# Later outputs, later normalisings and six turns in one group, in an mLSTM and mixture-of-experts kernel

## The chip, the cores and the metric

The kernel runs on one core of a Trainium2 chip. The metric is the device time of one execution in microseconds (us). Before the change it is 632.3 us, the median of three runs (631.77 to 632.38). The profiled execution took 632.11 us, of which the profile's span covers 630.3.

Names: PE is TensorE (matrix products), DVE is VectorE, ACT is ScalarE, POOL is GpSimd, SP is SyncE, which issues most of the DMAs. SBUF is the memory of the engines, PSUM the small one into which PE writes.

## The reference

Three stages in a row, all in fp32:

```python
# 1: mLSTM, batch 2, heads 8, sequence 768, head size 40 -> y (B,H,S,D)
m_new = max(f_gate + m, i_gate); f = exp(f_gate + m - m_new); i = exp(i_gate - m_new)
C = f*C + i*outer(v, k); n = f*n + i*k
y[t] = sigmoid(o_gate) * (C q) / max(|n.q|, 1)
# 2: four experts on x = y as (1536, 320), all of them for every token
out = sum_e p[:, e] * (relu(x @ w1[e]) @ w2[e])        # w1 320x1024, w2 1024x320
# 3: gated product
out = ((x @ w_a) * (x @ w_b)) @ w_out                  # 320x1536, 1536x320
```

## The kernel before, in words

**Stage 1** works in 12 units `u` of 128 tokens (6 chunks of time by 2 batches). For each unit PE multiplies queries and keys (`products`), reads the state (`from_state`), and multiplies the weighted scores with the values (`outputs`, 16 matmuls of 41 columns). DVE weighs the scores (`weigh`), scales the part from the state, takes the numerator out of PSUM (`take_num`), and normalises it: three operations on a tile `den` of 8 columns and one product into `normed` (`normalise`). POOL multiplies that with the output gate into `acc` (`gate_output`, which increments the semaphore `x_ready`). One bank holds the outputs of a unit, so `outputs(u)` waits until `take_num(u-1)` is done. In the last units PE also multiplies ones by ones (`keep_busy`), results of which nobody reads.

**Stages 2 and 3** work in 56 groups `n`. A group takes one pair of blocks of 128 hidden columns and one half of the tokens (768 of them). Its first layer is a two-by-two block product done with seven products instead of eight, on sums and differences of blocks of weights and of x (the operand of x has seven pieces, made of four quarters `raw` by four `x_sum` steps). Each product stands for fp32 as a high and a low part in a rounded format: PE issues four matmuls of 384 columns per product, high by high, high by low, low by high, and the remaining rows. ACT makes the high parts (`x_high`, `high_a`, `high_s`, `high_w2`, `high_hidden`), DVE the low parts by subtraction (`x_low`, `low_w2`, `low_relu`), POOL those of the weights. Groups 0 to 31 are the experts (eight groups an expert: four for one half of the tokens, four for the other), 32 to 55 the gated product.

Two PSUM banks, A and B, take the seven products in turn, so the steps of a group hang together: product 0 to A, `keep_p1` (ACT) copies it, product 1 to B, `make_c11` (DVE) adds the two; product 2, copied by `keep_u2`; product 3 needs c11 made; product 4, copied by `keep_w`; product 6 needs `make_c22` (B plus that copy); `make_c12` ends the group. PE fills in between with the second layer of the group before (36 matmuls of 320 columns in an expert's group, in portions given by `chunks`, the function `between` issues one portion after each product and each turn). The next group's product 0 waits for the second `low_relu` of this one, its product 1 for `make_c12`.

**Turning.** x is transposed by PE, 128 tokens at a time: six turns give one half of the tokens. Set 0 is turned during stage 1; sets 1, 2 and 3 (`BASES`, the group from which each is made ready) within groups. ACT first replicates a tail of 32 columns (`replicate`), PE turns `acc` and tail into bank B (`turn`), ACT copies the bank to `raw` (`keep_turned`), and only then can bank B be used again. When six are kept, the seven pieces of the operand are made (`x_high`, `x_low`, `x_sum`) for the half that starts at group 4, 32 or 36. Before, groups 1 and 2 turn three each for set 1, 29 and 30 for set 2, 33 and 34 for set 3.

**Order.** Each engine has its own written order and takes its instructions strictly in that order; semaphores hold an instruction until its inputs are there, and with it all behind it on its engine. Group 0 has no second layer to fill in, so there `between` issues the outputs of the last unit (half behind product 0, half behind product 1) and then 13 products with the identity (`keep_warm`).

Some tiles of the groups lie where tiles of stage 1 were. So ACT's `high_a(2)` and `high_a(3)`, the high parts of the third and fourth block of weights, wait until all twelve units have been gated:

```python
elif p >= 2:
    act.wait_ge(x_ready, NU)          # L633, in high_a
```

Of the kernel before, what the change touches and what calls it, by code (L numbers as in the profile page):

```python
# [26 lines left out]
P = 128  # L27
# [26 lines left out]
def mlstm_moe_kernel(nc, qk_t, tok, gates, late, probs, wt, wtail, w2, w_out, out):  # L54
    with ExitStack() as ctx:
# [159 lines left out]
        TURNS_AFTER = {0: (0,), 2: (1, 2)}  # L215

# [173 lines left out]
        def _(pool):  # L390
# [101 lines left out]
            for u in range(NU):  # L492
# [4 lines left out]
                if u >= 1:  # L497
                    sigmoid(u - 1)
                    gate_output(u - 1)
# [47 lines left out]
        def _(act):  # L547
# [231 lines left out]
            def keep_turn(n, k):  # L779

                if turning(n) is not None:
                    s, first = turning(n)
                    keep_turned(s, first + k, B_BANK)

            def expert_group(n):
# [7 lines left out]
                replicate_late(b2, 5)  # L793
                if b2 is not None:
                    x_high(b2, 0)
                high_c11(n)
                keep_u2(n)
                keep_turn(n, 1)
                keep_turn(n, 2)
                if b2 is not None:  # L800
                    x_high(b2, 1)
                if b3 is not None:
                    x_high(b3, 3)
# [5 lines left out]
                if n == 0:  # L809
                    prepare_weights(n)  # L810
                replicate_late(b1, 3)
                if b2 is not None:
                    x_high(b2, 2)
                if b3 is not None:
                    x_high(b3, 4)
# [5 lines left out]
                replicate_late(b1, 4)  # L821
                if b3 is not None:
                    x_high(b3, 5)
# [43 lines left out]
        def _(dve):  # L867
# [158 lines left out]
            for u in range(NU):  # L1026
# [5 lines left out]
                if u >= 1:  # L1032
# [3 lines left out]
                    normalise(u - 1)  # L1036
                if u >= 7:
                    x_low(0, u - 7)
                if u == 11:
                    low_w2(0)  # L1040
# [73 lines left out]
            def expert_group(n):  # L1114

                p = n % NP1
                b2, b3, b4 = (set_at(n, k) for k in (2, 3, 4))
                if p == 1:
                    add_tiles(n, range(HB, UB))
                if n == 0:  # L1120
                    x_low(0, 5)
                make_c11(n)
                if n == 0:
                    x_low(0, 6)
                    take_num(NU - 1)
                    normalise(NU - 1)
                low_relu(n, 0, c11_s[:, :])
# [366 lines left out]
```

## Time and profile before

| | before |
|---|---|
| median of three runs | 632.3 us (631.77 to 632.38) |
| the profiled execution | 632.11 us |
| its span | 630.3 us |
| PE busy in the span | 614.3 us (97%) |
| PE weight loads | 590.1 us (94%) |
| DVE busy | 375.2 us (60%) |
| ACT busy | 300.2 us (48%) |
| POOL busy | 221.6 us (35%) |
| mean granted clock of PE | 0.989 of full speed |

Stage 1 ends and group 0 begins at 79.00 us in the span; the gated groups begin at 424.79. "Idle before" in a row is the time for which the engine stood still ahead of an instruction, with the instruction that ended the wait. PE's matmuls overlap in the rows, so that the distance from start to start is what one costs. PEclk is the clock granted to PE, 1.00 for 2.4 GHz and 0.50 for 1.2 GHz; in a row of a longer stretch it is the mean.

### The profile page before, as it was taken

To read this page: it belongs to the slowest core of one execution; us is meant where nothing else is said; L and a number is where in the kernel's file an instruction comes from. 1 tells how busy PE (TensorE), PEld (TensorE's weight loads), DVE (VectorE), ACT (ScalarE), POOL (GpSimd) and SP (SyncE) were. 2 spreads that over 40 slices of the span, in tenths; PEclk is the share of its full clock that TensorE was granted. 3 is DMA by queue.
4 is the path that set the end of the run, shared out by engine and by line. 5 is a ranking of instruction groups with operands and counts; after the bars stand their busy time and mean duration, and the time that the engine had idled before them with its cause. 6 is when DMAs were issued, how large, how long until landed. Compare 5 with 4: busy or idle time off the path is not lost. (4 is left out here: it accounts for less than half of the span.)

```text
span 630.3 us, 11170 instructions
## 1 busy us (share of the span) xinstructions
PE 614.3 (97%) x4035; PEld 590.1 (94%) x4045; DVE 375.2 (60%) x714; ACT 300.2 (48%) x644; POOL 221.6 (35%) x289
## 2 busy tenths in 40 slices
PE   7999989999999999999999999999989999999997
PEld 6888889999999999999999999988779999999997
DVE  7577985685364353644444535387597564757565
ACT  4778645654444344443445434645644443444332
POOL 3468774032530033500435101364244640464000
PEclk9999959999999999999999999999999999999999
DMA  3667505102041002310022100113100420030011
GB/s 121 194 213 190 152 4 171 38 1 46 23 131 56 4 13 55 120 49 22 2 66 82 55 12 2 45 35 90 35 11 8 121 75 11 19 71 2 0 63 64
DMA packets 21063, 38.98 MB, mean 62 GB/s; under 512 B 3600, under 2 KB 11312, under 8 KB 21008
## 3 DMA queue, kind: packets, MB, share of 16 engines
q1 hardware_dynamic: 18976, 35.57, 20.1%
q10 hardware_dynamic: 2032, 2.68, 1.5%
q8 instruction: 33, 0.54, 0.4%
q14 instruction: 22, 0.18, 0.1%
HBM read 26.42 MB, written 1.97 MB: 45 GB/s over the span
## 5 line engine op out<-in xcount | busy, mean ns | idle before, releaser
L1386 PE MATMUL PS<-w2h,hh 128*128 128x320 f32 x528 | 164.5, 311 | 0.2
L1386 PE MATMUL PS<-w2l,hh 128*128 128x320 f32 x528 | 164.1, 311 | 0.0
L1386 PE MATMUL PS<-w2h,hl 128*128 128x320 f32 x528 | 163.2, 309 | 0.0
L1362 PE MATMUL PS<-xop,wop 128*128 128x384 f32 x392 | 139.2, 355 | 7.5 <-DVE xop L875 3.1
L670 ACT ACTIVATE hh<-c_s 128x384 fp32r<-128x384 f32 x144 | 75.3, 523 | 130.1 <-DVE c_s L1074 43.6
L1365 PE MATMUL PS<-xop,wop 96*128 96x384 f32 x392 | 133.0, 339 | 0.0
L1363 PE MATMUL PS<-xop,wop 128*128 128x384 f32 x392 | 132.8, 339 | 0.0
L1364 PE MATMUL PS<-xop,wop 128*128 128x384 f32 x392 | 132.7, 339 | 0.0
L1067 DVE TENSOR_TENSOR c_s<-PS,w_s 128x384 f32<-128x384 f32 x56 | 31.2, 558 | 122.9 <-ACT w_s L688 88.4
L1386 PEld LDWEIGHTS PS<-w2h,hh 128*128 128x128 f32 x528 | 99.5, 189 | 1.4 <-DVE hl L1051 1.2
L1386 PEld LDWEIGHTS PS<-w2l,hh 128*128 128x128 f32 x528 | 99.7, 189 | 0.0
L1386 PEld LDWEIGHTS PS<-w2h,hl 128*128 128x128 f32 x528 | 99.5, 188 | 0.0
L1362 PEld LDWEIGHTS PS<-xop,wop 128*128 128x128 f32 x392 | 74.2, 189 | 17.9 <-DVE xop L875 5.1
L452 POOL TENSOR_TENSOR wop<-s,wop 128x512 fp32r<-128x512 f32 x28 | 36.6, 1306 | 134.1 <-ACT wop L638 134.1
L1045 DVE SCALAR_TENSOR_TENSOR hl<-c_s,hh 128x384 fp32r<-128x384 f32 x96 | 56.2, 586 | 41.7 <-ACT hh L670 41.7
L1363 PEld LDWEIGHTS PS<-xop,wop 128*128 128x128 f32 x392 | 74.4, 190 | 0.0
L1365 PEld LDWEIGHTS PS<-xop,wop 96*128 96x128 f32 x392 | 74.2, 189 | 0.0
L1364 PEld LDWEIGHTS PS<-xop,wop 128*128 128x128 f32 x392 | 74.1, 189 | 0.0
L688 ACT ACTIVATE w_s<-PS 128x384 f32<-128x384 f32 x56 | 27.5, 491 | 80.5 <-PE PS L1365 80.4
L471 POOL TENSOR_TENSOR t1l<-t,t1h 128x384 fp32r<-128x384 f32 x7 | 7.1, 1019 | 115.1 <-ACT t1h L644 115.1
L1060 DVE TENSOR_TENSOR c_s<-PS,p_s 128x384 f32<-128x384 f32 x56 | 31.0, 554 | 21.3 <-PE PS L1365 21.1
L447 POOL TENSOR_TENSOR wop<-s,wop 128x384 fp32r<-128x384 f32 x28 | 29.5, 1052 | 39.8 <-ACT wop L634 39.8
(137 smaller groups left out, 866.0 us busy)
## 6 DMA issues: line engine op xcount, KB each, us to landing
wop<-t1h SPq DMA_DIRECT2D x56, 112.0 KB, 2.2
s<-in_wt SPq DMA_DIRECT2D x24, 256.0 KB, 3.0
kvo<-in_tok SPq DMA_DIRECT2D x12, 480.0 KB, 4.8
qk<-in_qk_t SPq DMA_DIRECT2D x24, 160.0 KB
s<-in_w SPq DMA_DIRECT2D x12, 320.0 KB, 3.0
wop<-t1l SPq DMA_DIRECT2D x28, 112.0 KB, 2.2
s<-in_w_out SPq DMA_DIRECT2D x12, 160.0 KB, 2.2
out_y<-acc SPq DMA_DIRECT2D x12, 160.0 KB, 1.9
```

The source lines that it names most:

```text
L447: nc.gpsimd.tensor_tensor(wop[p][:, 2, 0:3 * P], s1[:, p, P:4 * P], f32(wop[p][:, 0, 0:3 * P]), ALU.subtract).then_inc(w_lo_a, 1)
L452: nc.gpsimd.tensor_tensor(wop[p][:, 2, 3 * P:7 * P], s1[:, p, :], f32(wop[p][:, 0, 3 * P:7 * P]), ALU.subtract).then_inc(w_lo_s, 1)
L670: nc.scalar.activation(hh[:, home(n, k), :], src, ACT.Relu if n < FIRST else ACT.Copy).then_inc(hh_ready, 1)
L688: nc.scalar.activation(w_s[:, :], PS[:, A_BANK, 0:HT], ACT.Copy).then_inc(w_kept, 1)
L1045: nc.vector.scalar_tensor_tensor(out=hl[:, home(n, k), :], in0=src, scalar=0.0, in1=f32(hh[:, home(n, k), :]), op0=ALU.max, op1=ALU.subtra ...
L1060: nc.vector.tensor_tensor(c11_s[:, :], PS[:, B_BANK, 0:HT], p1_s[:, :], ALU.add).then_inc(c11_made, 1)
L1067: nc.vector.tensor_tensor(c22_s[:, :], PS[:, B_BANK, 0:HT], w_s[:, :], ALU.add).then_inc(c22_made, 1)
L1362: nc.tensor.matmul(bank, ws[0], xs[0], start=opens, stop=False, skip_group_check=True)
L1363: nc.tensor.matmul(bank, ws[0], xs[2], start=False, stop=False, skip_group_check=True)
L1364: nc.tensor.matmul(bank, ws[2], xs[0], start=False, stop=False, skip_group_check=True)
L1365: nc.tensor.matmul(bank, ws[1][0:96, :], xs[1][0:96, :], start=False, stop=closes, skip_group_check=True).then_inc(prod_done, 1)
L1386: got = nc.tensor.matmul(bank, left, (w2l if part == 1 else w2h)[p][:, f, :], start=opens and part == 0, stop=closes and part == 2)
```

## The change

Six edits, most of them to the order in which an engine has its instructions:

1. `keep_busy` in units 7 to 11 has two products of ones for three.
2. Group 0: both halves of the last unit's outputs now stand behind product 1. The identity products are ten for thirteen, go to another bank (`keep_fed`) and stand in portions of 2, 0, 1, 1, 2, 2, 2.
3. DVE: `normalise` of units 10 and 11 moves from ahead of the first `low_relu` of group 0 to the end of group 0, one ahead of `make_c12`, one behind it. The low parts 4, 5 and 6 of x stand together behind `make_c11`, `low_w2(0)` behind `make_c22`, `low_w2(1)` and the weights of the experts in group 1.
4. POOL: the x sum 2 moves from unit 10 to unit 9; the last two gates behind the sums and low parts of the second block of weights. ACT: `prepare_weights(0)`, which issues `high_a(2)`, moves to the end of group 0.
5. The six turns of set 1 are all in group 1, those of set 2 all in group 29: one behind product 0, five behind product 2. Set 3 stays as it was.
6. `x_high`, `x_low`, `x_sum` of sets 1 and 2 move about one group forward; the replication of the tails with them, in group 29 one ahead of `keep_u2` and two between kept turns.

```diff
+            for s in (1, 2):
+                if n == BASES[s] + 1:
+                    return s, 0, UB
             for part in range(2):
-                if set_at(n, part + 1) is not None:
-                    return set_at(n, part + 1), HB * part
+                if n == BASES[3] + 1 + part:
+                    return 3, HB * part, HB
...
+        def turns_behind(n, i):
+            if turning(n) is None or i not in (0, 2):
+                return ()
+            return (0,) if i == 0 else range(1, turning(n)[2])
...
-                return (3, 6, 1, 0, 6, 6, 1, 6, 4, 3) if n <= FIRST else (0, 5, 1, 0, 4, 4, 0, 3, 1, 0)
+                return (0, 5, 1, 0, 4, 5, 5, 4, 4, 1, 4, 1, 2) if n <= FIRST else (0, 5, 1, 0, 4, 4, 0, 3, 1, 0)
@@ POOL @@
-                    gate_output(u - 1)
+                    if u < NU - 1:
+                        gate_output(u - 1)
...
-                if u in (8, 9, 10):
+                if u in (8, 9):
                     x_sum(0, u - 8)
+                if u == 9:
+                    x_sum(0, 2)
                 if u == 10:
                     x_sum(0, 3)
+            sums(1)
             sigmoid(NU - 1)
-            sums(1)
+            low_s(1)
+            gate_output(NU - 2)
             gate_output(NU - 1)
-            low_s(1)
@@ ACT, expert_group @@
                 high_c11(n)
+                replicate_late(b1, 3)
                 keep_u2(n)
                 keep_turn(n, 1)
+                replicate_late(b1, 4)
                 keep_turn(n, 2)
...
+                replicate_late(b1, 5)
+                for k in range(3, UB):
+                    keep_turn(n, k)
...
                 keep_w(n)
-                if n == 0:
-                    prepare_weights(n)
...
                 replicate_late(b0, 1)
...
+                if n == 0:
+                    prepare_weights(n)
@@ DVE, units @@
-                    normalise(u - 1)
-                if u >= 7:
+                    if u < NU - 1:
+                        normalise(u - 1)
+                if 7 <= u < NU - 1:
                     x_low(0, u - 7)
@@ DVE, expert_group @@
                 low_relu(n, 2, c22_s[:, :])
+                if n == 0:
+                    normalise(NU - 2)
                 make_c12(n)
+                if n == 0:
+                    normalise(NU - 1)
                 low_relu(n, 3, c12_s[:, :])
@@ PE, between @@
-                    if slot < 2:
-                        outputs(NU - 1, (slot,))
+                    if slot == 1:
+                        outputs(NU - 1)
                     else:
-                        keep_warm((2, 3, 4, 2, 2)[slot - 2])
+                        keep_fed((2, 0, 1, 1, 2, 2, 2)[slot])
...
-                    keep_busy(3)
+                    keep_busy(2)
```

DVE in group 0, from the last low part of x (`xop0`) on; `num`, `den` and `normed` are the last units' tiles, `hl` the low parts of the hidden tile. Before:

```order
L874 TENSOR_TENSOR xop0<-raw,xop0 128x384 [waits x_hi]
L875 TENSOR_TENSOR xop0<-raw,xop0 32x384
L936 TENSOR_TENSOR num1<-PS,inter_s1 128x328 [waits inter_scaled,pv_done]
L944 SCALAR_TENSOR_TENSOR den1<-num1 128x8 [waits num_ready]
L946 TENSOR_SCALAR den1<-den1 128x8 [waits den_ready]
L948 RECIPROCAL den1<-den1 128x8 [waits den_ready]
L952 TENSOR_TENSOR normed1<-num1,den1 128x320 [waits den_ready,x_ready]
L1045 SCALAR_TENSOR_TENSOR hl<-c11_s,hh 128x384 [waits hh_ready]
L1067 TENSOR_TENSOR c22_s<-PS,w_s 128x384 [waits w_kept,prod_done]
L1045 SCALAR_TENSOR_TENSOR hl<-PS,hh 128x384 [waits hh_ready]
L1045 SCALAR_TENSOR_TENSOR hl<-c22_s,hh 128x384 [waits hh_ready]
```

And now, from `low_w2(0)` on:

```order
L903 TENSOR_TENSOR w2l0<-s2,w2h0 128x640 [waits w2_hi]
L1057 SCALAR_TENSOR_TENSOR hl<-PS,hh 128x384 [waits hh_ready]
L1057 SCALAR_TENSOR_TENSOR hl<-c22_s,hh 128x384 [waits hh_ready]
L957 SCALAR_TENSOR_TENSOR den0<-num0 128x8 [waits num_ready]
L959 TENSOR_SCALAR den0<-den0 128x8 [waits den_ready]
L961 RECIPROCAL den0<-den0 128x8 [waits den_ready]
L965 TENSOR_TENSOR normed0<-num0,den0 128x320 [waits den_ready,x_ready]
L1086 TENSOR_TENSOR c12_s<-PS,u2_s 128x384 [waits u2_kept,prod_done]
L957 SCALAR_TENSOR_TENSOR den1<-num1 128x8 [waits num_ready]
L959 TENSOR_SCALAR den1<-den1 128x8 [waits den_ready]
L961 RECIPROCAL den1<-den1 128x8 [waits den_ready]
L965 TENSOR_TENSOR normed1<-num1,den1 128x320 [waits den_ready,x_ready]
```

One normalising stood ahead of the first low part of `hl` (the other further up, in unit 11); now two stand around the c12 sum, behind the third.

ACT from group 0's `high_s(1)` (`wop1`) to group 1's first kept turn (`raw`); `wop2` is `high_a(2)`, `p1_s` is group 1's `keep_p1`. Before:

```order
L638 ACTIVATE wop1<-s1 128x512 [waits w_sum]
L688 ACTIVATE w_s<-PS 128x384 [waits prod_done]
L634 ACTIVATE wop2<-s1 128x384 [waits x_ready,w_in2]
L670 ACTIVATE hh<-PS 128x384 [waits prod_done]
L670 ACTIVATE hh<-c22_s 128x384 [waits c22_made]
L670 ACTIVATE hh<-c12_s 128x384 [waits c12_made]
L676 ACTIVATE p1_s<-PS 128x384 [waits c11_made,prod_done]
L583 ACTIVATE raw<-PS 128x2x2x128 [waits x_lo,xt_done]
```

And now:

```order
L649 ACTIVATE wop1<-s1 128x512 [waits w_sum]
L699 ACTIVATE w_s<-PS 128x384 [waits prod_done]
L681 ACTIVATE hh<-PS 128x384 [waits prod_done]
L681 ACTIVATE hh<-c22_s 128x384 [waits c22_made]
L681 ACTIVATE hh<-c12_s 128x384 [waits c12_made]
L645 ACTIVATE wop2<-s1 128x384 [waits x_ready,w_in2]
L687 ACTIVATE p1_s<-PS 128x384 [waits c11_made,prod_done]
L594 ACTIVATE raw<-PS 128x2x2x128 [waits x_lo,xt_done]
```

`high_a(2)`, with its wait for all twelve gates, moved from ahead of the group's last three high parts of `hh` to right ahead of group 1's `keep_p1` and kept turn.

## Rows read from the trace of the kernel before

**Rows 1.** Page, busy time by engine: us, share of the span, instructions.

```profile
PE 614.3 (97%) x4035; PEld 590.1 (94%) x4045; DVE 375.2 (60%) x714; ACT 300.2 (48%) x644; POOL 221.6 (35%) x289
```

**Rows 2.** Windows by stage: stretch, its length, busy us by engine, granted clock, DMA.

```profile
79.00:96.92 17.92, 16.04 (x73) 15.48 (x72) 14.11 (x25) 7.18 (x16) 14.02 (x17) 0.62 0.11 26
96.92:121.03 24.11, 24.10 (x156) 22.80 (x154) 14.26 (x26) 15.37 (x32) 6.74 (x8) 1.00 0.35 106
121.03:143.00 21.97, 21.16 (x130) 20.37 (x129) 18.57 (x32) 9.78 (x19) 5.79 (x7) 1.00 0.06 16
143.00:153.18 10.18, 10.18 (x66) 10.18 (x65) 5.05 (x11) 4.25 (x9) 4.12 (x6) 1.00 0.01 2
388.58:412.66 24.08, 24.05 (x154) 22.66 (x153) 12.07 (x22) 16.11 (x39) 7.72 (x10) 1.00 0.13 30
412.66:436.84 24.18, 21.46 (x131) 20.42 (x130) 19.54 (x31) 11.73 (x26) 11.80 (x13) 1.00 0.25 69
```

**Rows 3.** The same view by the microsecond, where the granted clock changes.

```profile
81.00:82.00 1.00, 0.91 (x5) 0.94 (x5) 0.97 (x2) 0.73 (x1) 1.00 (x2) 0.54 0.00 0
...
94.00:95.00 1.00, 1.00 (x7) 1.00 (x6) 0.37 (x1) 0.12 (x1) 1.00 (x2) 0.64 0.59 136
```

**Rows 4.** Timeline of PE: start, us, line, operation, count, idle before.

```profile
77.26 1.92 PE L1290 MATMUL PS<-vx,pt 128*128 128x41 f32 x16
...
79.00 0.42 PE L1362 MATMUL PS<-xop,wop 128*128 128x384 f32 x1
...
81.09 1.90 PE L1290 MATMUL PS<-vx,pt 128*128 128x41 f32 x8 [1.13 <-DVE num L936]
...
85.77 0.67 PE L1362 MATMUL PS<-xop,wop 128*128 128x384 f32 x1
...
89.00 0.66 PE L1362 MATMUL PS<-xop,wop 128*128 128x384 f32 x1 [0.75 <-DVE c_s L1060]
...
91.55 0.67 PE L1362 MATMUL PS<-xop,wop 128*128 128x384 f32 x1
```

**Rows 5.** Timeline of POOL, then of DVE, then of POOL again.

```profile
78.25 4.38 POOL L489 TENSOR_TENSOR raw<-raw 128x384 f32<-128x384 f32 x4
...
80.87 0.84 DVE L944 SCALAR_TENSOR_TENSOR den<-num 128x8 f32<-128x8 f32 x1
...
84.31 1.10 DVE L875 TENSOR_TENSOR xop<-raw,xop 32x384 fp32r<-32x384 f32 x1
...
90.68 0.17 DVE L944 SCALAR_TENSOR_TENSOR den<-num 128x8 f32<-128x8 f32 x1
...
91.97 1.12 POOL L441 TENSOR_TENSOR acc<-normed,ogate 128x320 f32<-128x320 f32 x1 [2.85 <-DVE normed L952]
...
98.85 0.82 DVE L890 TENSOR_TENSOR w2l<-s,w2h 128x640 fp32r<-128x640 f32 x1
```

**Rows 6.** Timeline of ACT, then the page's groups of instructions (busy, mean ns).

```profile
83.42 0.47 ACT L676 ACTIVATE p_s<-PS 128x384 f32<-128x384 f32 x1
...
L670 ACT ACTIVATE hh<-c_s 128x384 fp32r<-128x384 f32 x144 | 75.3, 523 | 130.1 <-DVE c_s L1074 43.6
...
L1045 DVE SCALAR_TENSOR_TENSOR hl<-c_s,hh 128x384 fp32r<-128x384 f32 x96 | 56.2, 586 | 41.7 <-ACT hh L670 41.7
```

**Rows 7.** Timeline of PE and ACT in group 1.

```profile
99.45 0.43 PE L1362 MATMUL PS<-xop,wop 128*128 128x384 f32 x1
...
102.60 0.33 PE L1206 MATMUL PS<-identf,acc 128*128 128x128 f32 x1
...
103.29 0.60 ACT L583 ACTIVATE raw<-PS 128x512 f32<-128x512 f32 x1 [0.74 <-PE PS L1208]
...
104.03 0.41 PE L1362 MATMUL PS<-xop,wop 128*128 128x384 f32 x1
```

**Rows 8.** Timeline of PE at groups 31 and 32, the longest pauses.

```profile
424.79 0.41 PE L1362 MATMUL PS<-xop,wop 128*128 128x384 f32 x1 [0.89 <-DVE hl L1045]
...
429.26 0.45 PE L1362 MATMUL PS<-xop,wop 128*128 128x384 f32 x1 [1.52 <-DVE xop L875]
```

More of the change, by code:

```diff
@@ L214, in mlstm_moe_kernel @@
         BASES = {1: 0, 2: FIRST - NP1, 3: FIRST}
-        TURNS_AFTER = {0: (0,), 2: (1, 2)}
         def set_at(n, k):
@@ L779, in keep_turn @@
             def keep_turn(n, k):
-                if turning(n) is not None:
-                    s, first = turning(n)
+                if turning(n) is not None and k < turning(n)[2]:
+                    s, first, _ = turning(n)
                     keep_turned(s, first + k, B_BANK)
@@ L820, in expert_group @@
                 replicate_late(b0, 1)
-                replicate_late(b1, 4)
-                if b3 is not None:
-                    x_high(b3, 5)
+                if b1 is not None:
+                    x_high(b1, 1)
+                if b2 is not None:
+                    x_high(b2, 4)
+                if n == 0:
+                    prepare_weights(n)
             def gated_group(n):
@@ L1116, in expert_group @@
                 p = n % NP1
-                b2, b3, b4 = (set_at(n, k) for k in (2, 3, 4))
+                b1, b2, b3, b4 = (set_at(n, k) for k in range(1, 5))
                 if p == 1:
                     add_tiles(n, range(HB, UB))
-                if n == 0:
-                    x_low(0, 5)
                 make_c11(n)
                 if n == 0:
-                    x_low(0, 6)
+                    for k in (4, 5, 6):
+                        x_low(0, k)
                     take_num(NU - 1)
-                    normalise(NU - 1)
                 low_relu(n, 0, c11_s[:, :])
+                if n == 1:
+                    low_w2(1)
                 if b2 is not None:
-                    x_low(b2, 0)
                     x_low(b2, 1)
+                    x_low(b2, 2)
+                    x_sum(b2, 0)
                 if b3 is not None:
-                    x_low(b3, 3)
-                    x_sum(b3, 1)
+                    x_sum(b3, 2)
+                    x_low(b3, 4)
                 if b4 is not None:
-                    x_low(b4, 5)
                     x_low(b4, 6)
@@ L1139, in expert_group @@
                     add_tiles(n, range(HB))
-                if b3 is not None:
-                    x_sum(b3, 2)
+                if n == 0:
+                    low_w2(0)
+                if b2 is not None:
+                    x_sum(b2, 1)
                 w2_lows(n)
@@ L1215, in keep_busy, with keep_fed @@
                     nc.tensor.matmul(PS[:, INTER, BUSY_COLS:BUSY_COLS + P], ones[:, :], ones[:, :], start=True, stop=True)
-            def keep_warm(n):
-                pe.wait_ge(inter_scaled, NU - B)
+            def keep_fed(n):
+                pe.wait_ge(state_ready, 2 * OLD)
                 for _ in range(n):
-                    nc.tensor.matmul(PS[:, INTER, BUSY_COLS:BUSY_COLS + P], identf[:, :], identf[:, :], start=True, stop=True)
+                    nc.tensor.matmul(PS[:, UPD, BUSY_COLS:BUSY_COLS + P], identf[:, :], identf[:, :], start=True, stop=True)
             def log_weights(u):
@@ L1338, in product @@
                 if turning(n) is not None and i == 1:
-                    s, first = turning(n)
+                    s, first, _ = turning(n)
                     pe.wait_ge(raw_ready, UB * s + first + 1)
@@ L1349, in product @@
                     if turning(n) is not None:
-                        s, first = turning(n)
-                        pe.wait_ge(raw_ready, UB * s + first + 3)
+                        s, first, count = turning(n)
+                        pe.wait_ge(raw_ready, UB * s + first + count)
                 elif i == 4:
@@ L1409, in turn_within @@
             def turn_within(n, k):
-                s, first = turning(n)
+                s, first, _ = turning(n)
                 if k == 0:
@@ L1451, in _ @@
                     slot += 1
-                    for k in TURNS_AFTER.get(i, ()) if turning(n) is not None else ():
+                    for k in turns_behind(n, i):
                         turn_within(n, k)
```

30 lines of the change are left out of this document (13 added, 17 removed).

## The prediction

> **What bounds the kernel now.** I read first the page's list of engines: TensorE is busy for 97% of the span [rows 1], so a change pays only where TensorE stands still, runs at the low clock, or gets less to do. Then the busy times by stage [rows 2]. A plain group of the experts takes 10.18 us. Five stretches hold what the change touches. Group 0 (79.00 to 96.92) takes 17.92 us at a mean granted clock of 0.62. Groups 1 and 2, with three turns each, take 24.11 together; groups 29 and 30 take 24.08. Against two plain groups (20.36) that is 3.7 us, 0.62 a turn, with TensorE never idle. Groups 3 and 4 take 21.97, so 1.6 are lost there; groups 31 and 32 take 24.18, so 3.8 are lost. The biggest pauses of the latter are 0.89 us (for the first low part of the hidden tile) and 1.52 us (for a low part of x) [rows 8].
>
> Next, the clock by the microsecond [rows 3]: it falls to its half level, 1.2 GHz, in the microsecond from 81 and is back at 2.4 GHz within the one from 94, some 13.6 us later. TensorE's own timeline [rows 4] shows what was before the fall: product 0 at 79.00, then a pause of 1.13 us for the last but one `take_num`. The second pause, 0.75 us, is ahead of product 3 at 89.00, and the clock rises 5.7 us after it.
>
> **The change, part by part, in the profiled execution's time (632.11 us, of which 630.3 are the span; the median is 632.3, 0.2 more).**
>
> *Ones and identity.* Five units lose one product of ones and group 0 has 10 identity products for 13. Only the one in unit 11 stands behind the last wait; I value it at 0.3 us earlier for product 0. The rest is filler in waits: nothing.
>
> *x sums.* GpSimd now does the third x sum in unit 9, right behind the second, ahead of unit 9's gate and so beside `normalise(9)`. In unit 11 of before, with four such sub-operations running from 78.25 for 4.38 us (1.1 each), the small den operation at 80.87 takes 0.84 us, and at 90.68, with GpSimd idle, 0.17 [rows 5]. Each ended when the GpSimd operation beside it ended. So `normalise(9)` and all that DVE does behind it in order, weigh, scale and `take_num(10)`, come 1.1 us later: `take_num(10)` ends at 81.95 for 80.84. The Trainium skill, "SBUF — State Buffer", section "SBUF: two separate sides", has this as a rule: an operation of VectorE with two inputs in SBUF and one of GpSimd take the shared port pair exclusively for the whole instruction. The trace agrees (0.84 against 0.17); were the port merely shared in width, this 1.1 us would be nearly nothing and the forecast 1 us lower.
>
> *Group 0.* Product 1 follows product 0 and ends about 80.9; the outputs wait for `take_num(10)` until 82.2, a pause of 1.3 us in place of 1.13. They then take 1.74 us (77.26 to 79.00 at the full clock [rows 4]). ACT's queue ahead of `keep_p1` is unchanged in length and ends its copy at 83.9 as before [rows 6]: unit 11's gates start 1.1 us later, but the wait for the last x sum is gone. DVE has the first c11 sum now ahead of the low parts 4, 5 and 6: c11 at 84.0 to 84.5, low part 4, with contention like the 1.10 us at 84.31 [rows 5], to 86.2. Product 2 waits for it until 86.4 (85.77 before), a second pause of over 2 us. So the clock falls here again. From 86.4 TensorE is never idle. By columns of the plain group (28 matmuls of 384 and 36 of 320 in 10.18 us) a product of four matmuls takes 0.70 us and a second-layer matmul 0.146; at half rate a product takes 1.4, and 89.00 to 91.55 [rows 4] leaves 0.4 for each of three identity products. Product 4 ends near 91.4 (91.55 + 1.4 = 93.0 before). If the clock rises 5.7 us after the pause, as in [rows 3, 4], that is at 92.1; group 0 ends at about 94.2 instead of 96.92. The pause ahead of product 3 is gone.
>
> *What is late next.* That gain of 2.7 us is, I think, lost at once. DVE now has, behind c22 and the low part of w2 (0.82 us with GpSimd idle, at 98.85), two low parts of 0.5, `normalise(10)`, the c12 sum, `normalise(11)`. A normalising is 1.2 us (90.68 to the gate at 91.97) [rows 5]. In numbers from 91.4 (durations overlap their neighbours by some 0.1): w copied 92.0; c22 92.6; w2 93.3; two low parts 94.4 (pitch from 586 ns each, the first waits for ACT, 523 ns [rows 6]); normalise 95.5; c12 96.0; normalise 97.4 (it meets the gate of unit 10); gate of unit 11, 1.12 us, 98.55 at best. ACT has `high_a(2)` at the end of group 0, which waits for all twelve gates, and behind it in order stand `keep_p1(1)` and the first kept turn of group 1. High part, copy and kept turn (0.45 + 0.4 + 0.6) end at 100.05. Product 1 of group 1 waits for that kept turn: 100.1 for 99.45 [rows 7]. Of the 6 us before it TensorE works 2: product 0, one turn (behind c12, 96.0) and five second-layer matmuls. **Cost 0.65 us**, with pauses of 1.3 and 2.8 us where there was none. Bounds: -0.5 (no contention on the port and an early rise) to +1.6.
>
> *Clock in group 1.* A pause of 1.13 us beside light work was enough at 81; a pause of 1.52 at 427.7, in dense work, was not (mean clock 1.00 in that stretch [rows 2, 8]). With 4 us idle of 6 I take the clock to fall. By the 5.7 us of before it is back at about 105.8, at the earliest near 103.5. In that time products 1 and 2 and the first turn run at half rate: 1.7 us of work to product 2's end twice over, and 0.3 to 0.5 of the first turn's interval. **Cost 2.0 us**; bounds 0 (no fall) and 2.9.
>
> *Six turns in one group.* All use bank B, so each waits until ACT has copied the one before: turn at 102.60, copy from 103.29 for 0.60, next at 104.03, an interval of 1.43 with six second-layer matmuls in it [rows 7]. With four or five in it, it would be 1.0 to 1.2 for TensorE, but the copy still holds it at 1.3 to 1.43; I take 1.37. Five such intervals are 6.85 us with 22 matmuls; before, the five hold 30 and take some 7.2. Eight matmuls (1.2 us) are owed for 0.35 saved. Ahead of product 1, where turn and copy bind, five stand for nine: 0.6 owed. Together 1.45, less 0.1 to 0.2 of switches between kinds: **1.3 us** at group 1, and 0.1 for a late low part at the end. At group 29 ACT in addition replicates a tail ahead of `keep_u2` and of the kept turn, which puts turn 2 0.4 us later: **1.75 us**. Bounds for both together 1.5 to 4.
>
> *A group earlier.* All six turned, the operand of the next half is split from group 2 (30) on. DVE's work between c11 and c22 of the group before its use falls from two low parts' and two sums' worth to one of each, and only low part 6 is left to the group of its use, whose sum GpSimd has by then. Its last wait moves behind product 4. I give back all of the 1.6 us of groups 3 and 4 and the 3.8 of 31 and 32: **-1.6 and -3.8**; bounds -0.6 and -2 (in groups 2 and 30 DVE gets two low parts, two sums and, in group 2, a w2 low part ahead of the low part on which the next group waits).
>
> *Sum.* 0.65 + 2.0 + 1.4 - 1.6 + 1.75 - 3.8 = +0.4 us. 632.1 + 0.4 = 632.5, on the median's footing **632.7 us**.
>
> **Rivals.** (1) *The clock holds in group 1*: for it, a pause of 1.52 did nothing at 427.7; against it, 1.13 sufficed at 81. Then 632.7 - 2.0 = 630.7. (2) *The chain over both normalisings is shorter*: no contention in units 9 and 11, so product 1 of group 1 comes at 99, the pause ahead is below 2 us and the clock stays: 632.7 - 1.1 - 2.0 = 629.6. (3) *The prepared operand does not come earlier where it counts*: DVE falls behind in groups 2 and 30, its operations lengthened beside GpSimd by up to 0.7 us each (0.84 for 0.17 [rows 5]), and the low part of the hidden tile holds product 0 of the next group. It decides once DVE needs over 7 us from c11 to that low part (product 1's end to the next product 0 is 8 us in a plain group, less 1 for c11 and ACT). Of the 5.4 given back 2.0 stay lost: 634.7, slower. For it: DVE is the releaser of both pauses shown. Against: it is busy 19.54 of 24.18 us there [rows 2], so the order binds and not its load.
>
> **How the numbers follow.** The likeliest, with its own range of 631.6 to 633.9, gets 0.47; rival 1 0.2; rival 2 0.1; rival 3, with a clock that stays low for longer (up to 2.9), 0.23. What a measurement can tell from no change is 0.2%, 1.3 us: under 631.0 or over 633.6. Faster: 0.2 + 0.1 = 0.30. Slower: 0.23 and a fifth of the likeliest, 0.32. Same: 0.38. Range: 629.8 to 635.2, which leaves out half of rival 2 and a tail of rival 3.
>
> **What would show it.** The outputs of unit 11 behind product 1 with 1.2 us or so idle ahead; product 2 at 86 to 86.5; group 0 ended by 94 to 95; DVE's two normalisings at 94 to 97.5; ACT waiting for the gate on GpSimd; product 1 of group 1 at 100; the clock low a second time from about 98 to 105; turns 1.3 to 1.45 us apart; groups 3, 4, 31 and 32 at 10.2 each. I am wrong if group 1 starts before 94 and its product 1 before 99, if the clock is 1.00 from 95 on, or if groups 31 and 32 together still take over 22 us.

## The result, and the profile after

The changed kernel takes **641.42 us** (median, 640.54 to 642.33, 4 runs), the kernel before beside it 632.34 us (631.77 to 633.45, 4 runs): ratio **1.0142, 95% interval 1.012 to 1.0163**. It is 9.1 us slower; forecast were 632.7 us and a range of 629.8 to 635.2. The profiled execution took 642.33 us, the longest of the four, with a span of 640.5: its stages below add up to 10.3 us, and what they share out is this one execution's difference, 1.2 us more than that of the medians.

The page's line of engines answers to [rows 1]: TensorE's busy time is the same (614.3 before), so the 10 us of the span are time in which it stands, 26.4 us for 16.0.

```profile
PE 614.1 (96%) x4019; PEld 587.9 (92%) x4029; DVE 374.1 (58%) x714; ACT 301.0 (47%) x644; POOL 220.5 (34%) x289
```

Windows by stage show where. The first five rows answer to [rows 2] stretch by stretch (group 0; 1 and 2; 3 and 4; 29 and 30; 31 and 32), the last three are single groups: 2, 29 and 30.

```profile
79.02:94.97 15.95, 12.15 (x66) 11.66 (x66) 10.85 (x19) 7.44 (x17) 8.20 (x10) 0.79 0.00 1
94.97:130.44 35.47, 28.13 (x155) 24.81 (x154) 18.93 (x38) 16.72 (x34) 10.85 (x14) 0.90 0.30 85
130.44:150.89 20.45, 20.45 (x128) 20.45 (x129) 15.75 (x28) 9.26 (x18) 5.57 (x7) 1.00 0.06 17
396.46:426.00 29.54, 25.39 (x154) 22.57 (x153) 15.33 (x25) 17.05 (x40) 10.34 (x12) 1.00 0.11 25
426.00:447.12 21.12, 20.98 (x130) 20.48 (x129) 16.71 (x27) 11.23 (x25) 9.67 (x10) 1.00 0.28 78
117.51:130.44 12.93, 11.06 (x64) 10.20 (x65) 11.42 (x21) 6.55 (x12) 2.14 (x3) 1.00 0.16 47
396.46:413.75 17.29, 14.70 (x90) 12.37 (x89) 4.45 (x10) 10.72 (x28) 3.85 (x6) 1.00 0.00 1
413.75:426.00 12.25, 10.70 (x64) 10.21 (x65) 10.88 (x16) 6.33 (x12) 6.48 (x7) 1.00 0.25 58
```

Group 0 gives 1.97 us, groups 3 and 4 give 1.52, groups 31 and 32 give 3.06. Groups 1 and 2 take 11.36 more (35.47 for 24.11) and groups 29 and 30 take 5.46 more (29.54 for 24.08). -1.97 + 11.36 - 1.52 + 5.46 - 3.06 = +10.3, and product 0 of group 33 stands at 447.12 for 436.84. Behind it, as in groups 5 to 28, nothing differs by more than 0.1 us.

**The first groups.** TensorE's timeline (start, us, line, operation, count, idle before), answering to [rows 4, 7]:

```profile
79.02 0.42 PE L1381 MATMUL PS<-xop,wop 128*128 128x384 f32 x1
...
82.71 1.95 PE L1309 MATMUL PS<-vx,pt 128*128 128x41 f32 x16 [1.58 <-DVE num L949]
86.87 0.69 PE L1381 MATMUL PS<-xop,wop 128*128 128x384 f32 x1 [2.21 <-DVE xop L888]
...
94.97 0.42 PE L1381 MATMUL PS<-xop,wop 128*128 128x384 f32 x1
...
97.05 0.30 PE L1225 MATMUL PS<-identf,acc 128*128 128x128 f32 x1 [1.13 <-DVE c_s L1086]
...
101.05 0.69 PE L1381 MATMUL PS<-xop,wop 128*128 128x384 f32 x1 [2.65 <-ACT raw L594]
```

The outputs (82.71) stand behind product 1 and wait 1.58 us for `take_num(10)`; product 2 (86.87) waits 2.21 us for a low part of x; group 0 ends at 94.97; and product 1 of group 1 comes at 101.05, 1.6 us later than before. In the mixed timeline of DVE, POOL and ACT ahead of it (answering to [rows 5, 6]) is the chain that the prediction named:

```profile
96.25 0.55 DVE L1086 TENSOR_TENSOR c_s<-PS,u_s 128x384 f32<-128x384 f32 x1
96.41 0.86 POOL L448 TENSOR_TENSOR acc<-normed,ogate 128x320 f32<-128x320 f32 x1 [5.12 <-DVE normed L965]
96.71 0.58 DVE L957 SCALAR_TENSOR_TENSOR den<-num 128x8 f32<-128x8 f32 x1
...
98.41 1.10 POOL L448 TENSOR_TENSOR acc<-normed,ogate 128x320 f32<-128x320 f32 x1 [1.15 <-DVE normed L965]
99.61 0.52 ACT L645 ACTIVATE wop<-s 128x384 fp32r<-128x384 f32 x1 [2.26 <-POOL acc L448]
100.04 0.47 ACT L687 ACTIVATE p_s<-PS 128x384 f32<-128x384 f32 x1
100.41 0.59 ACT L594 ACTIVATE raw<-PS 128x512 f32<-128x512 f32 x1
```

c12 (96.25), the last normalising, its gate (to 99.51), the high part that waits for it, product 1's copy and the first turn's, both queued behind that high part for order alone. Of the 6.08 us from group 1's start to its product 1 TensorE works 2.3 (the pauses are 1.13 and 2.65). The clock by the microsecond, answering to [rows 3], falls twice:

```profile
86.00:87.00 1.00, 0.13 (x1) 0.13 (x1) 0.94 (x3) 0.00 (x0) 0.00 (x0) 0.50 0.00 0
92.00:93.00 1.00, 1.00 (x6) 0.92 (x6) 0.44 (x1) 0.46 (x1) 0.00 (x0) 0.61 0.00 0
...
99.00:100.00 1.00, 0.00 (x0) 0.00 (x0) 0.00 (x0) 0.39 (x1) 0.52 (x1) 0.80 0.00 0
...
106.00:107.00 1.00, 0.17 (x1) 0.00 (x0) 0.45 (x1) 1.00 (x3) 0.00 (x0) 0.79 1.00 318
```

**Six turns.** The timeline of PE and ACT in group 29, from turn 0 to turn 2 (first instruction of each turn; the copies of turns 0 and 1):

```profile
397.79 0.30 PE L1225 MATMUL PS<-identf,acc 128*128 128x128 f32 x1 [0.47 <-ACT xrep L583]
398.45 0.60 ACT L594 ACTIVATE raw<-PS 128x512 f32<-128x512 f32 x1
400.76 0.30 PE L1225 MATMUL PS<-identf,acc 128*128 128x128 f32 x1
401.93 0.52 ACT L681 ACTIVATE hh<-c_s 128x384 fp32r<-128x384 f32 x1 [2.48 <-PE PS L1405]
402.76 0.47 ACT L693 ACTIVATE u_s<-PS 128x384 f32<-128x384 f32 x1
403.13 0.59 ACT L594 ACTIVATE raw<-PS 128x512 f32<-128x512 f32 x1
403.77 0.33 PE L1225 MATMUL PS<-identf,acc 128*128 128x128 f32 x1 [1.79 <-ACT raw L594]
```

Turn 2 comes 3.01 us behind turn 1, not 1.8: turn 1's copy is fourth in ACT's queue behind `high_c11`, and that waits until the second layer has read the tile it writes (L1405), which is 3 matmuls behind turn 1 now. In group 1 the interval is 3.39 us (104.05 to 107.44). In group 29 the other four intervals, from turn 2 to product 3, are 1.34 to 1.44, 5.47 us in all.

**The groups behind them.** DVE and POOL in group 30, from c11 to c22, and the product that waits:

```profile
418.75 0.55 DVE L887 TENSOR_TENSOR xop<-raw,xop 128x384 fp32r<-128x384 f32 x1
419.21 1.29 POOL L459 TENSOR_TENSOR wop<-s,wop 128x512 fp32r<-128x512 f32 x1 [5.20 <-ACT wop L649]
419.33 1.59 DVE L888 TENSOR_TENSOR xop<-raw,xop 32x384 fp32r<-32x384 f32 x1
...
420.95 1.27 DVE L887 TENSOR_TENSOR xop<-raw,xop 128x384 fp32r<-128x384 f32 x1
...
424.01 0.54 DVE L1079 TENSOR_TENSOR c_s<-PS,w_s 128x384 f32<-128x384 f32 x1
...
424.61 0.44 PE L1381 MATMUL PS<-xop,wop 128*128 128x384 f32 x1 [1.55 <-DVE c_s L1079]
```

A low part that takes 0.55 us alone takes up to 1.59 beside POOL's low parts of the weights. With two low parts, an x sum and that stretching between c11 and c22, c22 is late: product 6 of group 30 (the last row) stands still for 1.55 us.

### The profile page after: what moved, and what is told of

The parts are those of the page before. It is cut to its first block and busy times, and to the rows that moved or that the text cites. A ratio compares the mean times of both kernels' runs of the same rounds, so it can differ in the third digit from the quotient of the medians.

```text
span 640.5 us, 11132 instructions
## 1 busy us (share of the span) xinstructions
PE 614.1 (96%) x4019; PEld 587.9 (92%) x4029; DVE 374.1 (58%) x714; ACT 301.0 (47%) x644; POOL 220.5 (34%) x289
## 3 DMA queue, kind: packets, MB, share of 16 engines
HBM read 26.42 MB, written 1.97 MB: 44 GB/s over the span
## 5 line engine op out<-in xcount | busy, mean ns | idle before, releaser
L1405 PE MATMUL PS<-w2h,hh 128*128 128x320 f32 x528 | 165.2, 313 | 0.2 <-DVE hl L1063 0.2
L1405 PE MATMUL PS<-w2l,hh 128*128 128x320 f32 x528 | 163.8, 310 | 0.0
L1405 PE MATMUL PS<-w2h,hl 128*128 128x320 f32 x528 | 163.7, 310 | 0.0
L1405 PEld LDWEIGHTS PS<-w2h,hh 128*128 128x128 f32 x528 | 99.9, 189 | 1.3 <-DVE hl L1063 1.1
L1405 PEld LDWEIGHTS PS<-w2h,hl 128*128 128x128 f32 x528 | 99.8, 189 | 0.0
L1405 PEld LDWEIGHTS PS<-w2l,hh 128*128 128x128 f32 x528 | 99.8, 189 | 0.0
L1057 DVE SCALAR_TENSOR_TENSOR hl<-c_s,hh 128x384 fp32r<-128x384 f32 x96 | 54.8, 571 | 45.0 <-ACT hh L681 45.0
```

The lines of the kernel that those rows point to most:

```text
L1057: nc.vector.scalar_tensor_tensor(out=hl[:, home(n, k), :], in0=src, scalar=0.0, in1=f32(hh[:, home(n, k), :]), op0=ALU.max, op1=ALU.subtra ...
L1405: got = nc.tensor.matmul(bank, left, (w2l if part == 1 else w2h)[p][:, f, :], start=opens and part == 0, stop=closes and part == 2)
```

## The experiments

All times are medians of runs beside runs of the kernel before on the same chip. Group durations are from product 0 to product 0 in one profiled execution. TensorE's product 0 of group 0 stood between 78.8 and 85.3 us in them, in part for a reason told further down, so durations of groups can be compared and positions can't. Even a duration in group 0 is one execution's: the same code took 17.92 us there in one profile and 16.79 in another.

**first_group: the first group's edits alone**, three turns a group as before. Against the kernel before (its main lines):

```diff
-                    if slot < 2:
-                        outputs(NU - 1, (slot,))
+                    if slot == 1:
+                        outputs(NU - 1)
...
+                if u == 9:
+                    x_sum(0, 2)
...
+                if n == 0:
+                    prepare_weights(n)
```

> The first group's edits alone (outputs behind product 1, normalisings and gates late, the x sum in unit 9, the high part of the third weight block at the group's end), with three turns each in groups 1, 2, 29 and 30 as before. Theory A (most of the loss lies in the six turns of one group): group 0 takes 16 us for 17.9, product 1 of group 1 comes at 101 as in the changed kernel, the clock falls a second time, and the whole is 3 us above before, about 635.5; groups 29 to 36 as before. Theory B (most of the loss is the chain over normalisings, gate and high part at the start of group 1, with the clock): 638.5 or more.

Measured 634.87 us (634.70 to 637.79, 5 runs) against 632.76: ratio 1.0052 [1.0031, 1.0072], 2.1 us slower by the medians and 3.3 by the ratio (two of its five runs took over 637 us). Group 0 takes 14.93, groups 1 and 2 take 29.06 (24.11 before), groups 29 to 32 as before. Product 1 of group 1 waits 2.69 us for the same copy (row of PE), and the granted clock is low again from 103.9 to 107.3 us:

```profile
103.20 0.44 PE L1370 MATMUL PS<-xop,wop 128*128 128x384 f32 x1 [2.69 <-ACT raw L587]
```

So the part I thought a gain lost at once (+0.65 + 2.0 in my terms) is a loss of about that size by itself, as the first theory had it.

**six_turns: the six turns and the earlier x steps alone**, first group as before. Against the kernel before (its main lines):

```diff
-        TURNS_AFTER = {0: (0,), 2: (1, 2)}
...
+            return (0,) if i == 0 else range(1, turning(n)[2])
...
-                return (3, 6, 1, 0, 6, 6, 1, 6, 4, 3) if n <= FIRST else (0, 5, 1, 0, 4, 4, 0, 3, 1, 0)
+                return (0, 5, 1, 0, 4, 5, 5, 4, 4, 1, 4, 1, 2) if n <= FIRST else (0, 5, 1, 0, 4, 4, 0, 3, 1, 0)
```

> The six turns in one group and the x steps a group earlier alone; group 0 as before. Theory A: groups 29 and 30 together 29.5 us as in the changed kernel, 31 and 32 21.1, and the same shape at groups 1 to 4 (group 1 above 16.5, group 2 above 12), so 5 to 6 us above before, 637.5 to 638.5. Theory B: groups 1 and 2 lose only about what five copies cost, 2 us, and the whole is at 635 or below.

Measured 638.44 us (637.43 to 639.59, 4 runs) against 632.76: ratio 1.0091 [1.0074, 1.0108], 5.7 us slower. Windows of groups 1 and 2, 3 and 4, 29 and 30:

```profile
96.76:125.51 28.75, 25.75 (x156) 22.66 (x154) 16.63 (x30) 16.29 (x33) 7.08 (x9) 1.00 0.29 90
125.51:145.95 20.44, 20.44 (x129) 20.44 (x130) 15.74 (x28) 9.26 (x18) 5.56 (x7) 1.00 0.06 17
391.52:421.06 29.54, 25.39 (x155) 22.57 (x153) 15.33 (x25) 17.05 (x40) 10.31 (x12) 1.00 0.11 25
```

Against [rows 2]: 4.6 more, 1.5 less, 5.5 more; groups 31 and 32 take 21.11 (3.1 less). Group 1 takes 16.81 and group 2 takes 11.94: with the clock up, 2.9 us are lost in the six turns (16.81 + 10.18 - 24.11) and 1.8 in group 2. It is the larger half. By the medians the two halves add up to 7.8 of 9.1 us, by the ratios to 1.43% of 1.42%, so the times don't show that anything is left over. The profiles show one place where the two halves meet. In group 2 of the changed kernel DVE has the experts' weights (four small operations, 0.98 us) ahead of the low part of x and of c11; here it had them in group 1. Product 3 comes 4.90 us behind the group's start for 4.34 here, product 6 10.77 for 9.78, and that is the 1.0 us by which the group is longer (12.93 for 11.94).

**nine_ahead: three matmuls of the second layer more ahead of turn 1's product**, so that `high_c11` finds its tile read.

```diff
-                return (0, 5, 1, 0, 4, 5, 5, 4, 4, 1, 4, 1, 2) if n <= FIRST else (0, 5, 1, 0, 4, 4, 0, 3, 1, 0)
+                return (0, 5, 1, 3, 4, 4, 4, 4, 3, 1, 4, 1, 2) if n <= FIRST else (0, 5, 1, 0, 4, 4, 0, 3, 1, 0)
```

> The changed kernel with three of the second-layer matmuls moved from behind turns 1 to 5 to between product 2 and turn 1 (portions 0,5,1,3,4,4,4,4,3,1,4,1,2), so that all nine that read the hidden tile's first slot are issued before turn 1. Theory A says that ACT's first high part of the group waits for these nine, with the copy of turn 1 behind it: the interval from turn 1 to turn 2 falls from 3.0 to 1.8 us in group 29 and from 3.4 to 2.2 or less in group 1; 2 to 3 us less than the changed kernel, 638.5 to 639.5. Theory B (the interval is the copy's length and ACT's replication alone): no change, 641.4.

Measured 641.13 us (640.12 to 642.65, 4 runs): ratio 1.0135 [1.0117, 1.0153], no difference that can be told from the changed kernel. The wait did go, as the rows of group 29 show (turn 1, `high_c11`, turn 2):

```profile
400.19 0.27 PE L1225 MATMUL PS<-identf,acc 128*128 128x128 f32 x1
...
400.45 0.53 ACT L681 ACTIVATE hh<-c_s 128x384 fp32r<-128x384 f32 x1 [2.01 <-PE PS L1405]
...
402.29 0.33 PE L1225 MATMUL PS<-identf,acc 128*128 128x128 f32 x1 [0.92 <-ACT raw L594]
```

Turn 2 stands 2.10 us behind turn 1 for 3.01, in group 1 it is 1.83 for 3.39; but group 29 takes 16.82 for 17.29. The account: turn 1 itself is 0.44 later, since three matmuls (3 x 0.146) stand ahead of it, and the four later intervals still take 5.47 us in all, now with 15 matmuls in them for 18. A turn takes 0.41 and each filler 0.146, so in the changed kernel 2.0 us stand empty in the interval of 3.01 and 1.2 in the four others (5.47 - 4 x 0.41 - 18 x 0.146); here 1.1 and 1.6, 2.7 in all. A group of six turns has 36 such matmuls and six copies' worth of waits: moving fillers empties another place. My expectation of 2 to 3 us was wrong. What is gained is the 0.47 us between 3.2 and 2.7 in group 29 and 0.8 in group 1 (21.72 for 22.54), so the wait of `high_c11` alone is not the price of the six turns.

**late_high: the weights' high part behind the first copy of group 1.**

```diff
                 keep_turn(n, 0)
+                if n == 1:
+                    prepare_weights(0)
...
-                if n == 0:
-                    prepare_weights(n)
```

> The changed kernel with the high part of the third weight block issued behind group 1's first kept turn instead of ahead of it and of the copy of product 0. Theory A (that wait for the last gate holds group 1's product 1): product 1 starts at 98.4 instead of 101.05, the pause ahead of it falls from 2.65 us to nearly none; 2.5 us less, 639, and if the clock then holds, 2 us less again, 637. Theory B (ACT is held by something else, the c12 sum or the gates elsewhere): no change, 641.4.

Measured 637.09 us (637.06 to 637.98, 5 runs): ratio 1.0073 [1.0059, 1.0087], 4.3 us below the changed kernel. Product 1 of group 1 and the high part, then the windows of groups 1 and 2:

```profile
97.72 0.44 PE L1381 MATMUL PS<-xop,wop 128*128 128x384 f32 x1
...
99.00 0.53 ACT L645 ACTIVATE wop<-s 128x384 fp32r<-128x384 f32 x1 [1.32 <-POOL acc L448]
```

```profile
94.34:112.04 17.70, 14.76 (x91) 12.45 (x90) 7.77 (x18) 10.26 (x22) 9.48 (x12) 1.00 0.48 135
112.04:124.97 12.93, 11.07 (x64) 10.20 (x65) 11.43 (x21) 6.54 (x12) 2.15 (x3) 1.00 0.16 47
```

Product 1 stands 3.38 us behind group 1's start for 6.08: 2.70 for the queue on ACT. Group 1 takes 17.70 for 22.54. I put the other 2.14 down to the clock, which is 1.00 in the whole group here and was low for 6.8 us there; I had 2.0. The price is that of one execution: in the profile of after_three, further down, the clock is low for half as long (102.1 to 105.5) and group 1 takes 21.91, which leaves 1.5.

**pool_after: POOL's low parts of the weights in groups 2 and 30 wait for DVE's first x sum**, so that they don't run beside DVE's work ahead of c22.

```diff
+                if i == 3:
+                    pool.wait_ge(t_sum, 4 * 1 + 1)
                 low_s(i)
...
+                if set_at(n, 2) == 2:
+                    pool.wait_ge(t_sum, 4 * 2 + 1)
```

> The changed kernel; in groups 2 and 30 GpSimd waits, before it makes the low part of a weight block, until VectorE has made the low parts 1 and 2 and the first sum of x. Theory A2 (groups 2 and 30 are 2.7 and 2.1 us over a plain group because VectorE and GpSimd hold each other up between c11 and c22): VectorE's low parts there take 0.55 us an operation again for up to 1.59, group 30 falls from 12.25 to 10.7 or less and group 2 from 12.9 to 11.5; 2.5 to 3 us less, 638.5. Rival (VectorE's order alone, too much work between c11 and c22): groups 2 and 30 as before, 641.4.

Measured 643.67 us (641.29 to 645.69, 4 runs) against 632.77: ratio 1.017 [1.0143, 1.0197], 2.3 us above the changed kernel for 3 below it, a miss. Groups 30 and 31, and a low part of DVE in group 30:

```profile
416.55:427.54 10.99, 10.59 (x64) 10.20 (x64) 9.62 (x16) 6.33 (x12) 2.88 (x3) 1.00 0.28 65
427.54:438.94 11.40, 10.93 (x65) 10.31 (x65) 10.09 (x14) 6.08 (x12) 7.29 (x11) 1.00 0.13 30
```

```profile
422.12 0.55 DVE L892 TENSOR_TENSOR xop<-raw,xop 32x384 fp32r<-32x384 f32 x1
```

The low parts are back at 0.55 us and group 30 at 10.99 for 12.25: the hold-up on each other was what made c22 late. But 0.81 of the 1.26 us come back in group 31, where POOL's work now runs. In group 2 the same move shows inside one group: product 6 comes 9.74 us behind its start for 10.77, but POOL now runs beside the second x sum (1.80 us for 0.95), the low parts behind it are late, the next product 0 waits 1.46 us for one of them, and the group takes 12.74 for 12.93 where I expected 11.5. The whole is no faster; in its profile the clock was low for some 13 us in the last units (64 to 77), ahead of anything that this edit touches.

**six_mended: the last three edits together.**

```diff
+                if n == 1:
+                    prepare_weights(0)
...
+                return (0, 5, 1, 3, 4, 4, 4, 4, 3, 1, 4, 1, 2) if n <= FIRST else (0, 5, 1, 0, 4, 4, 0, 3, 1, 0)
...
+                    pool.wait_ge(t_sum, 4 * 2 + 1)
```

> All three mendings on the changed kernel: the high part of the third weight block behind group 1's first kept turn, nine second-layer matmuls ahead of turn 1, GpSimd's low part behind VectorE's in groups 2 and 30. If their gains add: 637.1 less 0.4 less 2.7, 634.0, so still above before, because six copies in one group cost 1.34 us each where PE has too little second layer to fill them. Rival (the gains overlap): 636.

Measured 636.25 us (635.24 to 639.66, 6 runs): ratio 1.0061 [1.0037, 1.0085]. 5.2 below the changed kernel, 3.5 above the one before, and the rival's time, not the sum of the expected gains. Groups 1 and 2 take 29.99, 5.9 more than before; groups 29 and 30 take 27.80, still 3.7 more than before, 31 and 32 take 21.91, 2.3 less. Six turns in one group stay a loss with every wait that I found taken away.

**first_late: the first group's edits with late_high's, three turns.** Against first_group:

```diff
                 keep_turn(n, 0)
+                if n == 1:
+                    prepare_weights(0)
...
-                if n == 0:
-                    prepare_weights(n)
```

> The first group's edits with three turns each as before, and the high part of the third weight block behind group 1's first kept turn. Theory A: the chain over both normalisings and the gates is off ACT's way, product 1 of group 1 starts at about 98, the clock does not fall a second time; 4.3 us less than the first group's edits alone, as with six turns: 630.5, 2 us faster than before. Rival (the gain was that of the six-turn group, with three turns the c12 sum or the copies bind): 633 or more.

Measured 632.52 us (631.44 to 634.27, 12 runs): ratio 0.9997 [0.9985, 1.0009], the kernel before's time. It is 2.3 us below first_group by the medians, and 2 us above what I expected; why, stays open. In the profile group 0 takes 14.82 and groups 1 and 2 take 25.85, 1.35 less than before together, but product 0 of group 0 stood at 82.40.

**first_late_pool: the same with waits for POOL in groups 3 and 31.**

```diff
+                if set_at(n, 3) == 2:
+                    pool.wait_ge(t_sum, 4 * 2 + 3)
...
+                    pool.wait_ge(x_lo, 14 * set_at(n, 3) + 10)
                     x_sum(set_at(n, 3), 3)
```

> The kernel first_late, and in group 31 GpSimd waits for VectorE's last x sum before it makes low parts, and in groups 3 and 31 its own x sum waits for the low part 4. If the two engines' mutual hold-ups made part of the 3.8 us lost in groups 31 and 32 of before: 1.5 to 2.5 us less there, 628.5. Rival (the waits only move GpSimd's work under the next operations of VectorE, and its x sum comes later than it is needed): no gain or 1 us more, 630.5 to 631.5.

Measured 634.11 us (631.30 to 638.56, 12 runs): ratio 1.002 [1.0002, 1.0039]. Against first_late group 31 falls from 12.23 to 10.65 and group 32 rises from 12.04 to 12.84; groups 3 and 4 take 25.09 for 21.97, at a mean clock of 0.93. Most of that is one pause in group 4, ahead of a product that waits for a low part of x:

```profile
139.62 0.45 PE L1373 MATMUL PS<-xop,wop 128*128 128x384 f32 x1 [2.53 <-DVE xop L882]
```

The clock is low right behind it, from 140.1 to 143.6. The work that waits is late in the next group. A miss.

**before_two, first_late_three, after_three: two products of ones per late unit against three.** Three profiles of kernels with two had shown a low clock in the late units, so I suspected the edit I had valued at nothing.

```diff
-                    keep_busy(3)
+                    keep_busy(2)
```

(first in the kernel before, undone in first_late and in the changed kernel)

> The kernel before with one edit: two products of ones per late unit instead of three. Theory A (the third product does nothing, as the forecast had it): the time is that of the kernel before within 0.2% (ratio 0.999 to 1.001), and executions spread as widely as before's (631.3 to 634.2). Theory B (the third product holds the clock in the late units: in the profiled executions of three kernels with two products the granted clock fell to 0.50 within the units 6 to 12, between 63 and 77 us, and product 0 of group 0 came at 82.2, 82.4 and 85.3 instead of 79.0): the median rises by 1 to 3 us (ratio 1.0015 to 1.005), some executions are 3 us or more above the lowest, and a profiled one of those shows the clock at 0.50 somewhere between 60 and 80 us.

> The first group's edits with the weights of group 2 prepared behind group 1's first copy (three turns as before), and three products of ones per late unit, as the kernel before has them. Theory A (the third product does nothing): 632.5, as with two. Theory B (it holds the clock in the late units): product 0 of group 0 at 79.0 to 79.5 in every profile, groups 0 and 1 take 14.8 and 13.8, so that group 2 starts at 107.7 against 108.97 before; median 630.5 to 631.3, ratio 0.997 to 0.999, faster than the kernel before.

> The changed kernel with three products of ones per late unit. Theory A: 641.4, no difference from the changed kernel. Theory B: its profile had product 0 of group 0 at 79.0, so its median can fall only by the executions in which the clock fell in the units: 0 to 1 us, 640.5 to 641.4; the spread gets narrower.

Measured: before_two 633.22 us (631.10 to 635.15, 12 runs), ratio 1.0002 [0.9988, 1.0015]; first_late_three 632.38 (631.16 to 635.56, 12 runs), ratio 0.9997 [0.9983, 1.0011]; after_three 642.42 (641.13 to 642.88, 4 runs), ratio 1.0147 [1.0131, 1.0163]. The third product does nothing that these medians can show, as forecast. In before_two's profile the clock is low from 76 us, behind a pause of 1.27, and in first_late_three's it is not, so the third product may matter in single executions; two more profiles don't settle that, and the medians show no price. The profiles show instead one reason why product 0 of group 0 wanders. The first matmul recorded behind the transfer of the decay rows, in first_late_three, then in the kernel before:

```profile
12.38 0.38 PE L1245 MATMUL PS<-mask,identb 128*128 128x512 bf16 x1 [1.34 <-DMA dec_r<-llo]
```

```profile
10.77 0.59 PE L1238 MATMUL PS<-dec_r,dec_l 66*128 66x512 f32 x1 [0.37 <-DMA dec_r<-llo]
```

The last of these transfers is issued at 10.14 us in one and 10.15 in the other, with the same code there, and what waits for it starts 1.6 us later. That is 1.6 of the 2.7 us by which product 0 of group 0 is later in first_late_three (81.72 for 79.00). first_late_three has groups 0 to 2 in 40.77 us (42.03 before) and the same median; a gain of 1.3 us in one profile each is not confirmed by 12 and 23 runs (0.17% at most by the interval's lower end, 1.1 us), and before_two's group 0, the same code as before's, took 16.79 for 17.92. No version here beats the kernel before.

## Why the prediction was wrong

By its own terms, from the groups' durations (before and after have group 0 at 79.00 and 79.02):

| Term | forecast | measured |
|---|---|---|
| Group 0 shorter | -2.7 | -1.97 |
| Group 1's start to its product 1 | +3.4 | +3.55 |
| Clock in group 1 | +2.0 | +2.14 (by late_high, what is left of group 1) |
| Six turns in group 1 | +1.4 | +2.9 (what is left; six_turns: 2.9) |
| Group 2 behind them | 0 | +2.75 |
| Groups 3 and 4 | -1.6 | -1.52 |
| Six turns in group 29 | +1.75 | +3.39 |
| Group 30 behind them | 0 | +2.07 |
| Groups 31 and 32 | -3.8 | -3.06 |
| Sum | +0.4 | +10.3 |

"Six turns" are counted here with group 2 and group 30 at a plain 10.18 us; what these two take above it stands in its own row. The sum is the profiled execution's; the medians differ by 9.1.

- **The first group was right in its chain.** Outputs behind product 1 with a pause (1.58 for 1.3), product 2 at 86.87 (86.4), group 0 ended at 94.97 (94.2), the chain over two normalisings, gate, high part and copies, product 1 at 101.05 (100.1), the clock low a second time from 99 to 106 (98 to 105). The x sum beside DVE's work on unit 9 cost 1.6 us (82.71 less 79.02, against 2.09 in six_turns), forecast 1.1; `normalise(9)` alone takes 2.64 us for 1.27. The experiments bear out the two costs, 2.70 by the queue and 2.14 by the clock, though the second came out so near in part by luck, since another execution gives 1.5.
- **Two steps failed, and the larger is in "A group earlier": groups 2 and 30 stood at nothing in the sum and cost 4.8 us (2.75 + 2.07).** The step was right where it gives (groups 3 and 4 give 1.52 of 1.6, groups 31 and 32 give 3.06 of 3.8) and wrong where it takes, though I had written into its bounds that DVE gets more in groups 2 and 30. With them the two places give +1.23 and -0.99, outside the bounds of -0.6 and -2. That was rival 3, priced at 2.0. Its condition was right, but mostly another product waits than it had: product 6, for c22. Its argument against (DVE 19.54 of 24.18 busy, so the order binds) was no argument: after, DVE is busy 10.88 of 12.25 in group 30, and its operations are long because POOL runs beside them. pool_after shows that this is the cause in group 30, and that most of it moves rather than goes. In group 2, 1.8 of the 2.75 are there with the first group as before (six_turns); the other 1.0 comes with the experts' weights, which edit 3 put ahead of c11 there; the two traces show it, and no run moved them alone.
- **The second is "Six turns in one group"**, at 1.4 + 1.75 with bounds of 1.5 to 4 for both places; they cost 6.3. I took 1.37 us for all five intervals from one row of a turn with six matmuls in it. For four of the five in group 29 that was right (5.47 us for 5.48). The one behind turn 1 is 3.01, and that is the whole miss of 1.64 there; in group 1 it is 3.39. I had gone through the bank's copies but not through ACT's queue, where `high_c11`, ahead of the copy, waits for the second layer to have read its tile. nine_ahead shows that sizing this wait was not all: with it gone only 0.47 us of group 29 come back, because the three matmuls moved ahead of it are missing behind the later turns. There are too few fillers for six copies.
- The range was too narrow because both of these costs were named and bounded by the nearest row, and both lay outside.

The Trainium skill, "SBUF — State Buffer", section "SBUF: two separate sides", says that VectorE with two inputs in SBUF and GpSimd lock each other out for a whole instruction. Here the trace agrees again: the low part that starts 0.12 us behind a POOL operation of 1.29 us takes 1.59 and ends 0.42 behind it, and takes 0.55 with POOL held back.

## What to carry to other kernels

When steps are packed into one stage, count the work that is left to fill their waits, and walk the queue of the engine that serves them, with what each entry waits for, before using the interval seen when they were spread. When work is moved ahead to relieve a stage, price the stage that receives it with operations stretched by its neighbours, not at their length when alone. A step put behind a late result must not stand in a queue ahead of work that does not need it: moving one high part by two places gave back 4.3 us (2.3 with three turns a group).

## What the runs showed of the hardware

- A short pause in light work (in or next to the late units' matmuls of 41 and 128 columns) can bring the low clock where a longer one in dense work (384 and 320 columns) does not. Behind 1.13 us in group 0 of the kernel before the clock was low from 81.1, within 1.00 us in the units of first_late from 74.0; but it was 1.00 throughout groups 29 to 32 of the changed kernel, with pauses of 1.79 and 1.55 us. Dense work is no protection from a longer one: in first_late_pool 2.53 us in group 4 were followed by the low clock. Nor does a pause decide it by itself: behind 1.27 us at the same place in the units the clock was low from 76.1 in before_two, and stayed at 1.00 until 84.8 in six_mended.
- A group 0 that runs at the low level for 12.1 of its 14.82 us (mean 0.59, in first_late) is no longer than one at 0.77 in first_group (14.93). In the first TensorE is busy for 14.77 us and never waits; in the second it is busy for 11.71 and waits for DVE. So the higher mean clock of the second bought no shorter group here.
- With the transfers at the start issued at the same time, the matmul that waits for them started 1.6 us later in one execution than in another; over all thirteen profiles it stands between 10.7 and 12.4 us. A difference of 1 us at one place in one profile is below that.
